# Attention, routed experts and a feed-forward layer in one kernel: routing of three batches moved into attention, gates stored beside x, filler matmuls in the gap

## The reference, cut to what matters

```python
x = attention(q, k, v).transpose(0, 2, 1, 3).reshape(3072, 512)
logits = x @ w_gate + modality_bias[modality_id]     # 3072 x 8
e_idx = argmax(logits, axis=1)
gate_w = softmax(logits)[arange(N), e_idx]
for e in range(8):
    mask = e_idx == e
    out[mask] = gate_w[mask, None] * (relu(x[mask] @ w1[e]) @ w2[e])   # 512 -> 1024 -> 512
h = out @ w_in                                       # 512 -> 2048
return (h * sigmoid(1.702 * h)) @ w_out
```

## Time and profile before

| what | value |
|---|---|
| median of three runs | 1146.36 us |
| the profiled execution | 1148.82 us |
| its span, first to last instruction | 1146.6 us |
| TensorE busy | 1103.9 us, 96% of the span |
| VectorE busy | 429.7 us, 37% |
| ScalarE busy | 376.8 us, 33% |
| POOL busy | 299.9 us, 26% |
| mean granted clock of TensorE | 0.979 |

### The profile page before, as it was taken

The page is one execution under the profiler, slowest core; times in us unless marked ns, Lnnn a source line. Parts: engine busy times, 40 slices in busy tenths (PEclk is TensorE's granted clock), DMA queues, the critical chain, the costliest instruction groups (busy, mean ns, idle before and its releaser), DMA issues.

```text
span 1146.6 us, 18452 instructions
## 1 busy us (share of the span) xinstructions
PE 1103.9 (96%) x5844; PEld 933.2 (81%) x5845; DVE 429.7 (37%) x1109; ACT 376.8 (33%) x780; POOL 299.9 (26%) x394
## 2 busy tenths in 40 slices
PE   9999999926999999999999999999999999999998
PEld 9999999915888888888887888888888888888887
DVE  5666656685222224222265223323223222222222
ACT  3666666613222233212254222222222222222222
POOL 8888889202662212212110001001001001000100
PEclk9999999956999999999999999999999999999999
DMA  9999998136111115211133001101000100000000
GB/s 221 229 247 238 234 239 224 47 102 242 37 37 55 37 46 192 67 53 46 37 107 123 19 1 46 27 0 46 18 9 37 27 9 19 18 0 0 37 1 37
DMA packets 57390, 92.01 MB, mean 80 GB/s; under 512 B 7936, under 2 KB 32768, under 8 KB 57344
## 3 DMA queue, kind: packets, MB, share of 16 engines
q1 hardware_dynamic: 51584, 72.56, 23.7%
q0 software_dynamic: 5760, 18.89, 4.8%
HBM read 72.02 MB, written 19.41 MB: 80 GB/s over the span
## 4 chain that ended last, share of the span: by engine, by line
PE 92%; DVE 4%; issue 1%; ACT 1%; POOL 1%; DVEq 0%; ACTq 0%; POOLq 0%
PE psum L837 8%; PE psum L828 8%; PE psum L830 8%; PE psum L839 8%; PE psum L829 8%; PE psum L838 8%; PE psum L686 6%; PE psum L770 4%; PE psum L771 4%; PE psum L772 4%; PE psum L795 4%; PE psum L797 4%; PE psum L796 4%; PE psum L661 3%; PE psum L649 2%; PE psum L782 2%
## 5 line engine op out<-in xcount | busy, mean ns | idle before, releaser
L1421 DVE TENSOR_TENSOR g<-psum,g 128x512 f32<-128x512 f32 x96 | 66.3, 691 | 306.5 <-ACT g L1024 306.4
L1024 ACT ACTIVATE g<-psum 128x512 f32<-128x512 f32 x96 | 57.5, 599 | 319.0 <-PE psum L830 316.1
L828 PE MATMUL psum<-x2T,win_hi 128*128 (+1 forms) x384 | 153.1, 399 | 2.3 <-DVE g L1421 2.3
L837 PE MATMUL psum<-w_hi,gT_hi 128*128 128x512 f32 x384 | 153.2, 399 | 0.0
L830 PE MATMUL psum<-x2T,win_lo 128*128 (+1 forms) x384 | 152.5, 397 | 0.0
L829 PE MATMUL psum<-x2T,win_hi 128*128 (+1 forms) x384 | 152.0, 396 | 0.0
L839 PE MATMUL psum<-w_hi,gT_lo 128*128 128x512 f32 x384 | 150.4, 392 | 0.0
L838 PE MATMUL psum<-w_lo,gT_hi 128*128 128x512 f32 x384 | 149.3, 389 | 0.0
L618 POOL DMA_INDIRECT out<-o_out,out_rows x20 | 19.5, 976 | 424.3 <-ACT o_out L1037 419.7
L686 PE MATMUL psum<-v_sb,pT 128*128 128x73 f32 x704 | 106.0, 269 | 1.7
L1148 DVE CUSTOM_DVE_ANT_0 s_msk<-psum,mask_sb 128x260 f32<-128x260 f32 (+1 forms) x192 | 74.8, 403 | 74.1 <-PE psum L650 38.9
(11 more groups left out here) (200 smaller groups left out, 1950.7 us busy)
## 6 DMA issues: line engine op xcount, KB each, us to landing
qk_raw<-qkT SPq DMA_DIRECT2D x64, 384.0 KB, 9.2
stage<-w SPq DMA_DIRECT2D x12, 1024.0 KB, 6.1
x<-y_rows SPq DMA_DIRECT2D x24, 256.5 KB, 2.6
vT_sb<-vT SPq DMA_DIRECT2D x16, 384.0 KB, 10.4
v_sb<-vP SPq DMA_DIRECT2D x16, 384.0 KB
x_rows<-x_sb SPq DMA_DIRECT2D x16, 384.0 KB, 8.0
win_raw<-w_in SPq DMA_DIRECT2D x16, 256.0 KB, 10.3
stage<-w_out SPq DMA_DIRECT2D x4, 1024.0 KB, 6.5
```

What stands on the lines that cost most here:

```text
L828: pe.matmul(bank, wh, hi, start=(c == 0), stop=False)
L837: pe.matmul(psum[:, OB[t], :], gh, hi, start=(f == 0), stop=False)
L1421: dve.tensor_tensor(g32[:, f % 2, :], psum[:, FB[f % 2], :], g32[:, f % 2, :], ALU.mult)\
```

## The change

- The routing of batch b - 1 is done in pieces inside batch b, for b = 1 to 3 (`route` on VectorE, with `choose`, `shift`, `make_gates`, `count_tiles`, `take_ranks`, `whole_tiles`, `rows_in_tile`, `mark_rows`; `rank_tiles` on TensorE in step 17; `gate_exps` on ScalarE in step 9). Each batch carries on the counts of the one before (`seen`). The biases are picked in batch 0.
- The logits of seven heads are added in the last step, the eighth's behind its last values (`add_heads`, `add_last_head`).
- After the last batch the same is done for its 6 tiles alone. TensorE counts in eight small matmuls, among them the tokens per expert. The first expert's number is sent to SyncE ahead of the table (`first_e`, `expert_known`). The base of each expert is added behind the ranks.
- `oh_slot` holds the token's number, and the 24 inverse matmuls are 32 columns wide, where they were 96.
- Gates go to memory as a 513th column of x_rows (`store_gates`, per batch 768 pieces of four bytes) and come back with the gathered rows; VectorE copies them out (`gates`). POOL waits for the last gates ahead of its first gather.
- The gather list is written straight from PSUM; the first three gathers use it without a copy; the table and the scatter list are made behind it.
- ScalarE and VectorE split the first expert's weights in quarters, with the first slot's halves between them. The first `up` doesn't wait for the table.
- `keep_going` puts 8, 16 and 16 small matmuls on ident behind the last values, behind the counts and behind the inverse.

```diff
@@ SyncE
+            def store_gates(b):
+                sp.wait_ge(gates_made, b + 1)
+                rows = x_dram.rearrange("(b t p) n -> b p t n", b=B, p=P)[b]
+                sp.dma_start(rows[:, :, DM:XW], gate[:, b * QT:(b + 1) * QT].rearrange("p (t o) -> p t o", o=1),
+                             allow_slow_non_contiguous=True)\
+                  .then_inc(gates_stored, 16)
...
                     store_pair(b, c)
+                    if b and c == 1:
+                        store_gates(b - 1)
+                    if b == B - 1 and c == PAIRS - 1:
+                        store_gates(b)
...
+            sp.wait_ge(expert_known, 1)
+            load_run(0, sp.value_load(first_e[0:1, 0:1], min_val=0, max_val=E - 1))
             sp.wait_ge(runs_ready, 1)
...
-            load_run(0, sp.value_load(table[0:1, RUN_E:RUN_E + 1], min_val=0, max_val=E - 1))
@@ POOL
             for c in range(PAIRS):
                 pool.wait_ge(x_stored[c], DMA * B + DMA)
+            pool.wait_ge(gates_stored, B * 16)
             pool.wait_ge(tables_ready, 1)
...
+                pool.wait_ge(gate_taken, t + PRIMED)
...
-            total = pool.value_load(table[0:1, TOTAL:TOTAL + 1], min_val=NTILE - 4, max_val=SLOTS - 4) + 4
             for t in range(3):
                 gather(t)
+            pool.wait_ge(runs_ready, 1)
+            total = pool.value_load(table[0:1, TOTAL:TOTAL + 1], min_val=NTILE - 4, max_val=SLOTS - 4) + 4
@@ TensorE
+            def rank_tiles(b):
+                pe.wait_ge(onehot_ready, b + 1)
+                pe.wait_ge(vw_moved, 2 * ((b + 1) * PAIRS + RANK_PAIR + 1))
+                pe.wait_ge(consts_made, 6)
+                at, tiles = psum[:, VW_ps, RANK_AT:RANK_AT + QT * E], slice(b * QT, (b + 1) * QT)
+                pe.matmul(at, tri[:], onehot[:, tiles, :].rearrange("p t e -> p (t e)"), start=True, stop=False)
+                pe.matmul(at, ones[:], seen[:, tiles, :].rearrange("p t e -> p (t e)"), start=False, stop=True)\
+                    .then_inc(ranks_ready, 1)
...
+            def keep_going(times):
+                for _ in range(4 * times):
+                    pe.matmul(psum[:, XB, 0:P], ident[:], ident[:], start=True, stop=True)
+
+            pe.wait_ge(scores_masked, B * HT + AHEAD)
+            keep_going(2)
+
+            pe.wait_ge(onehot_ready, B)
...
+            mm.then_inc(ranks_ready, 1)
+            keep_going(4)
...
-                mm = pe.matmul(psum[:, 2, 0:3 * SLOTS], oh_slot[:, t, :], oh_val[:, t].rearrange("p a s -> p (a s)"),
+                if t >= last_b:
+                    pe.wait_ge(ohs_ready, t - last_b + 2)
+                mm = pe.matmul(psum[:, 2, 0:SLOTS], oh_slot[:, t, :], tile_eq[:, t, :],
                                start=(t == 0), stop=(t == NTILE - 1))
+            mm.then_inc(ohs_used, 1)
+            keep_going(4)
@@ VectorE
+            def route(b, n):
+                if n == 6:
+                    choose(b)
+                if n == 7:
+                    shift(b)
+                if n == 11:
+                    make_gates(b)
+                if n == 12:
+                    count_tiles(b, range(0, QT // 2))
+                if n == 13:
+                    count_tiles(b, range(QT // 2, QT))
+                    dve.sem_inc(onehot_ready, 1)
+                if n == RANK_STEP + 2:
+                    take_ranks(b)
+                if n == RANK_STEP + 6:
+                    whole_tiles(of(b))
+                    rows_in_tile(b)
+                for k in range(QT // 2):
+                    if n == MARK_STEP + 6 * k:
+                        then(mark_rows(b * QT + 2 * k))
+                        then(mark_rows(b * QT + 2 * k + 1))
...
+                if b and n < HT:
+                    route(b - 1, n)
...
+            choose(B - 1)
+            dve.sem_inc(onehot_ready, 1)
+            shift(B - 1)
+            scale_head(B - 1, H - 1)
+            make_gates(B - 1)
...
+            first_low(0, w1_high, w1_split)
             xs_low(0)
+            first_low(1, w1_high, w1_split)
+            for c in range(PAIRS):
+                dve.wait_ge(x_stored[c], DMA * B + DMA)
+            first_low(2, w2_high, w2_split)
             xs_low(1)
+            first_low(3, w2_high, w2_split)
+            make_scatter()
+            dve.wait_ge(runs_ready, 1)
```

More of the change, by code:

```diff
@@ L943, in step, with gate_exps @@
                     spread_sinks(b, n // (2 * QT))
[L945 to L955 removed]
+                if b and n == EXP_STEP:
+                    gate_exps(b - 1)
+            def gate_exps(b):
+                act.wait_ge(shifted, b + 1)
+                if b:
+                    act.wait_ge(gates_made, b)
+                act.activation(exps_of[:], below[:], ACT.Exp).then_inc(exped, 1)
+            each_step(step)
+            gate_exps(B - 1)
             def run_and_first(t):
@@ new lines, in _ @@
+            sq = [P, E, E]
+            e_col = iota_row[:, 0:E].rearrange("p (s o) -> p s o", o=1).broadcast_to(sq)
+            e_row = iota_row[:, 0:E].rearrange("p (o e) -> p o e", o=1).broadcast_to(sq)
+            then(dve.tensor_tensor(lower[:], e_col, e_row, ALU.is_gt))
+            then(dve.tensor_scalar(seen[:, 0, :], from_end[:], 0.0, None, ALU.mult))
+            then(dve.tensor_copy(tri[:], tri_f[:]))
+            then(dve.tensor_copy(ones[:], ones_f[:]))
+            full, some = [P, NTILE, E], [P, QT, E]
@@ new lines, in choose, with shift @@
+            def choose(b):
+                then(dve.tensor_tensor(tied[:], lg[:, of(b), :], col(best[:], some), ALU.is_equal))
+                then(dve.tensor_tensor(tied[:], tied[:], row(from_end[:], some), ALU.mult))
+                then(dve.tensor_reduce(lead[:], tied[:], AX.X, ALU.max))
+                then(dve.tensor_tensor(onehot[:, of(b), :], tied[:], col(lead[:], some), ALU.is_equal))
+            def shift(b):
+                dve.tensor_tensor(below[:], lg[:, of(b), :], col(best[:], some), ALU.subtract).then_inc(shifted, 1)
@@ L1256, in _ @@
-            then(dve.tensor_copy(runs_before, busy))
-            both = e_cnt[:, 3:6:2, :]
-            for e in range(1, E):
-                then(dve.tensor_tensor(both[:, :, e:e + 1], both[:, :, e:e + 1], both[:, :, e - 1:e], ALU.add))
+            choose(B - 1)
[3 more added lines that the diff above has]
+            make_gates(B - 1)
+            count, tiles, tend = ranks_ps[:, QT, :], rank_t[:, NTILE:NTILE + E], e_cnt[:, 3, :]
@@ L1261, in _ @@
+            mark_slots(slice(0, (B - 1) * QT)).then_inc(ohs_ready, 1)
+            then(mark_slots(slice((B - 1) * QT, NTILE)))
+            rows_in_tile(B - 1)
+            for t in range((B - 1) * QT, NTILE):
+                mark_rows(t).then_inc(ohs_ready, 1)
+            busy, runs_before = e_cnt[:, 4, :], e_cnt[:, 5, :]
+            then(dve.tensor_tensor(tend, base_e[:], tiles, ALU.add))
+            then(dve.tensor_scalar(busy, tiles, 0.0, None, ALU.is_gt))
             tab = [P, SLOTS, E]
```

384 lines of the change are left out of this document (206 added, 178 removed).

## The result

The changed kernel takes 1211.01 us (median of four runs, 1205.25 to 1220.14), the kernel before 1147.59 in the same session. The ratio is 1.0561 (95% interval 1.0488 to 1.0633): **slower by 5.6%**. The forecast was 1130.4, with a range of 1123 to 1136.

A forecast was written before the change was run, and what follows sets the result against it. The prediction took TensorE to bound the kernel except in one hole, a serial VectorE chain after attention. Its terms, -19.5 + 2.3 + 0.6 + 0.6 = -16.0 us against a median of 1146.36, gave 1130.4 us, range 1123 to 1136.

The forecast's parts named there:

- Inside attention: Attention, batches 1 to 3: 17.8 us of added VectorE routing work costed at nothing, hidden in VectorE's idle time.
- The sign that the prediction named for being wrong: Attention, batches 1 to 3: a pair of heads longer than 13.7 us would show the forecast wrong.
- The added VectorE work is not hidden: Rival, attention: a third of the 17.8 us exposed gives 1136, all of it 1148, no gain; chance 0.09.
- The start: Kernel start: five serial VectorE operations ahead of the first mask delay TensorE's third score pair, +0.6 us (0 to 1.1).
- The gap: Last head's logits to the expert matmuls: shorter VectorE chain and gather, first expert matmul -19.5 us, later stall +2.3.
- Gather list: End of VectorE's chain after the last head's logits: list ready at 242.5 us, 18.7 earlier than 261.21.
- the fourth rival: Gate store holds POOL's first gather, kernel gets slower: up to +26.1 us, 1156.5; chance 0.03.
- undisturbed: Rival, first gather: it comes through undisturbed by weight loads, -2.5 us and faster matmuls, 1126 to 1128; chance 0.18.
- First expert matmul: After the first gather lands: transposes, xsT_hi and xsT_lo take 2.7 us, so it starts at 252.2 against 271.71, -19.5.
- the second rival: Fillers do not hold TensorE's clock ahead of the gather list: together +2 us, 1132.4; chance 0.10.
- Stall ahead of the first down matmul: First expert slot: 6.85 us of VectorE work ahead of hT_lo, 4.5 of it covered, +2.3 us (0 to 3).
- The rank matmuls' +0.6: Attention: TensorE's two rank matmuls of 48 columns per batch are not hidden, 0.2 us per batch, +0.6 (0.3 to 1.5).

The follow-up runs named there:

- GpSimd's pieces: The changed kernel with each of GpSimd's two long subtractions per head cut into six of 128 columns: 1161.27 us, ratio 1.0113.
- PSUM operands: The changed kernel with one input or the output of each VectorE routing operation of batches 0 to 2 in PSUM: 1167.67 us, ratio 1.0182.
- the work spread: The kernel with PSUM operands, routing spread to at most two, once three, small operations behind one mask, old addresses behind xs: 1143.78 us, ratio 0.9974.

## Why the prediction was wrong, step by step

**The step that failed** is "Inside attention": "I cost it at nothing. The cover is in the rows". In place of nothing stood +66.5 us, and 60 operations of that kind alone cost 58. VectorE did have idle time, but idle time was not what the added operations needed: those with two SBUF inputs, or TENSOR_SCALAR from SBUF to SBUF, also wait for GpSimd's current instruction. The cover was argued from the bias block of the earlier trace rows, which lies between 214 and 217 us. GpSimd's last split in the kernel before ended at 206.6, and from there to the end of attention it is idle:

```profile
206.34 0.23 POOL L554 TENSOR_TENSOR k_lo<-qk_raw,k_hi 128x24 fp32r<-128x24 f32 x1
```

The comparison was thus made in the one part of attention where nothing could hold VectorE. In batches 1 to 3 GpSimd is busy for most of the time (158.54 of 206.53 us from the first head to the last, and idle at the end), and the same kind of operation costs up to nine times its length there. The durations themselves (0.21 for 48 columns) were right wherever GpSimd was idle, as the gap shows. The sign that the prediction named for being wrong appeared: pairs of heads, 13.5 us before, took up to 23.8 in batches 1 to 3.

The rival that named the place ("The added VectorE work is not hidden") had the right place with the wrong price: "all of it 1148" took the plain durations as the most that could be lost. The bound of a cost must not stop at the operation's own length when another engine can hold it. And it had one term where a late mask cost twice: TensorE waited, and then worked at a lower clock (33.4 and 33.1 us of the 66.5).

**The start** was forecast at +0.6 (0 to 1.1) and became +5.1. Two of its five small operations were held as well, by subtractions of GpSimd from 12.86 to 14.67 and from 14.74 to 16.54; the chain of work that ended last shows them:

```profile
12.90 1.86 DVE lower L1202
14.78 1.80 DVE seen L1203
```

That is 3.2 more than the 0.4 to 0.5 of two such operations; TensorE then had to wait for the masks behind them.

**The gap** was right in nearly every step. Of the changed kernel, VectorE:

```profile
302.77 0.21 DVE L1340 TENSOR_TENSOR lg_parts<-psum,rden 128x48 f32<-128x48 f32 x1
303.01 0.21 DVE L1236 TENSOR_TENSOR lg<-lg,lg_parts 128x48 f32<-128x48 f32 x1
...
313.32 0.19 DVE L1442 TENSOR_SCALAR gather_i<-psum 128x32 int32<-128x32 f32 x1
```

The chain of work that ended last has the store of the gates and the first gather between them (start us, us until landed):

```profile
306.00 7.91 DMA x_rows<-gate
315.10 6.70 DMA xs<-x_rows,gather_i
```

TensorE:

```profile
305.45 3.82 PE L786 MATMUL psum<-ident 128*128 128x128 f32 x32
...
312.79 6.53 PE L786 MATMUL psum<-ident 128*128 128x128 f32 x32
321.85 1.10 PE L824 MATMUL psum<-ident,xs 128*128 128x128 f32 x4 [2.54 <-DMA xs<-x_rows,gather_i]
324.36 0.80 PE L839 MATMUL psum<-w_hi,xsT_hi 128*128 128x512 f32 x1 [1.40 <-DVE xsT_lo L1514]
...
343.32 0.50 PE L864 MATMUL psum<-w_hi,hT_hi 128*128 128x512 f32 x1 [2.77 <-DVE hT_lo L1522]
```

- *Gather list*: 10.74 us from the last logits (L1340 at 302.77, the twin of L1170, to 313.51); forecast 11.05.
- *Gate store and the first gather*: the store of the last gates was forecast to land 3.5 us ahead of the list. It took 7.91 and landed at 313.91, 0.4 behind the list. So the mechanism of the fourth rival is there, at a few tenths of a us; what made this store long was not tried. The gather started 1.6 after the list (forecast 0.9) and landed 6.70 later (forecast 6.1, bounds 3.57 to 7.1): "undisturbed" falls.
- *First expert matmul*: 2.56 after the landing (forecast 2.7); in all 21.59 us from the last logits where it was 40.26, **-18.7** against the forecast -19.5.
- *Fillers*: the first sets run at the full clock (32 in 3.82 us), the last one at the lower level in good part (32 in 6.53, mean clock 0.57 from 312.8 to 319.4). So the second rival is there in part, without a price at the list: the inverse was done at 312.95, and the list, on VectorE's own chain, began at 313.32. The expert's first 24 matmuls, kept at 8.46, took 7.66.
- *Stall ahead of the first down matmul*: 2.77, forecast 2.3.

Together -16.3 from L1340 on, where the terms gave -17.2. Two readings in the prediction are slightly off without changing it: the second gather's issue was 1.02 us longer (2.17 against 1.15), not 1.2, and the scatter list took 3.89, not 3.85. The rank matmuls' +0.6 cannot be told apart in the trace.

**The expert loop** had no term in the sum. Its +5.1 comes from a tile that became one word wider, an edit for which the sum had no price at all.

The range was right for the gap alone; the chances gave 0.03 to a slower kernel, all of it to the gate store.

## What to carry to other kernels

Before idle time of VectorE is counted as cover, look at what GpSimd runs in those same microseconds: an operation with two SBUF inputs, or a TENSOR_SCALAR from SBUF to SBUF, can last until GpSimd's current instruction ends, and a serial chain of them pays at each step. An operand in PSUM, a reduction, shorter GpSimd instructions, or a stretch in which GpSimd is idle avoid it; then keep what remains to one or two operations behind each mask. And a row that serves as proof of cover must come from the stretch where the new work will run.

## What was not expected of the hardware

- A VectorE operation of 6 columns took 1.80 us (L1282), a GpSimd subtraction's length; 60 operations of 0.2 us cost 58 us so, and 4.5 us as reductions.
- In the changed kernel, waits of TensorE cost about as much again through its clock: the mean granted clock was 0.87 and 0.83 in batches 1 and 2, with 12 us of idle time in each. Neither the sum of the waits nor the longest one settles it: from 30 to 230 us TensorE was idle for 12.9 us with GpSimd's pieces, 12.6 with PSUM operands and 11.3 with the work spread, no wait lasted longer than 1.6, and the mean clock was 0.98, 0.93 and 1.00. What decides between them is not shown.
- The expert loop, bound by TensorE, runs 1.7% slower (12.49 to 12.51 against 12.28 us per slot) when the tiles behind `xs` lie 32 or 64 bytes from their old place, and not when they lie 2048 bytes from it.
